# One block for every stage of an attention, cosine-layer and gated-layer kernel, with bias tiles copied straight from the staging buffer

## The chip, the cores and the metric

The kernel runs on one core of a Trainium2 chip. The metric is the device time of one execution in microseconds (us). Before the change it is 1207.83 us, the median of three runs from 1207.55 to 1208.03. The core's engines run their own instruction streams and meet at semaphores: PE (TensorE, matmuls; its weight loads are shown as PEld), DVE (VectorE), ACT (ScalarE), POOL (GpSimd) and SP (SyncE), which here only starts DMA transfers.

## The reference

```python
# attention over (batch 4, heads 8, seq 576, head_dim 64)
scores = q @ k.T / sqrt(64)
x = (log1p(|i - j|) / log1p(max(i, 1)))[..., None]
bias = relu(x @ w1 + b1) @ w2          # hidden 32, one value per head
attn = softmax(scores + bias);  a = attn @ v
x = a.transpose(0, 2, 1, 3).reshape(2304, 512)
h = x @ w_in;  x = (h * cos(h)) @ w_out                  # d_ff 2048
xn = x / sqrt(mean(x * x) + 1e-6) * rms_g
out = (silu(xn @ w_gate) * (xn @ w_val)) @ w_out2         # d_ff 1536
```

All data are float32. The bias depends on the position and the head only, so it is computed once (8 x 576 x 576) and used by all four batches.

## The kernel before

The program has four stages, and each is a `with nc.Block() as block:` of its own. At the end of a block all engines meet before any of them starts the next block.

**Bias stage** (`bias_phase`, lines 71 to 281). There are 12 rounds (`N`), and a round makes 3 groups (`KINDS`) of 16 rows for all 8 heads. ACT and DVE make the hidden values, PE multiplies them into the banks `bias_ps`, ACT writes the result into one of two sets of staging buffers (line 183, `stage_out`), and SP stores each group to a scratch tensor in DRAM (line 148). After 10 rounds SP loads the first three bias tiles of attention back from there (line 323). The staging of a later round waits until the store of the round two before it has landed.

**Attention stage** (`attention_phase`). There are 16 pairs of heads, numbered 0 to 15 here. A pair has 10 tiles of queries, five for each of its two heads, called s0 to s9; s4 and s9 have 64 rows, the others 128. One bias tile is held for each s; a new set is loaded every four pairs. In a slot PE makes the scores of a tile (line 506), turns an earlier tile (lines 528 and 532) and at slots 3, 5, 8 and 0 runs a quarter of the mix with the values (lines 546 and 552). The scores of a tile wait for the DVE's result on the tile two before it. DVE adds the bias and takes the maximum (line 644), ACT takes the exponential (line 594) and copies turned tiles, DVE and POOL share the normalising (line 412), and POOL splits q and k of the next pair in a high and a low part. In the last pair POOL splits the weight units 0 to 2 of the next layer in its place, and units 3 to 7 after it (lines 777 and 782). At the stage's start SP loads the other seven bias tiles. At its end PE runs the mix of pair 15's first half, then the first chunk `first_h` of the cosine layer, whose inputs DVE and ACT split just then (`features.high`, `features.low`, lines 803 to 812), and then the mix of the second half.

**Cosine layer** (`cos_layer_phase`). Six tiles of 384 tokens, each with 16 chunks f. An `up` and a `down` are 12 matmuls each; `down(f)` follows `up(f+2)`. The chain of a chunk is: ACT line 1080 (`turns`), DVE lines 1116, 1121 and 1126, ACT line 1094 (sine), DVE line 1133 (product), ACT line 1066 (high part), POOL line 1184 (low part). In the first tile DVE and POOL also split two weight units per chunk, of f = 0 to 11, beginning with units 8 and 9. These go to the space that attention's tensors had. At the stage's start POOL sets constants, among them an identity matrix.

**Gated layer** (`gated_layer_phase`). Again six tiles, with 12 chunks of two `up` and one `down`. Its first gate and value are made at the end of the cosine layer.

Every engine runs its stream in order, so an instruction that waits holds back all that stands behind it.

Of the kernel before, what the change touches and what calls it, by code (L numbers as in the profile page):

```python
# [35 lines left out]
EARLY_TILES = 3  # L36

# [4 lines left out]
LAG1, LAG2 = 3, 2  # L42
UNIT = KC * P
# [27 lines left out]
def bias_phase(nc, sb, sem_of, ins, bias_scratch, att):  # L71
# [36 lines left out]
    bias_staged = [sem_of(f"p0_bias_staged{k}") for k in range(KINDS)]  # L108
    bias_stored = att.bias_stored
# [7 lines left out]
    assert N % 2 == 0 and EARLY % 2 == 0  # L117
# [10 lines left out]
    with nc.Block() as block:  # L128

        @block.sync  # L130
        def _(sp):
            sp.dma_start(table[:, :], ins["log_table"]).then_inc(table_in, 16)
            sp.dma_start(inv_psi[:, :], ins["inv_psi"]).then_inc(consts_in, 16)
            sp.dma_start(w1b1[:, :], ins["w1b1"]).then_inc(consts_in, 16)
            sp.dma_start(w2rep[:, :], ins["w2rep"]).then_inc(w2_in, 16)
            sp.wait_ge(w2_zero, 1)
            for g in range(GR):
                sp.dma_start(w2blk[g * HID:(g + 1) * HID, g, :], ins["w2"]).then_inc(w2_in, 16)
            for h in range(2):
                att.load_qk(sp, 0, h, True)  # L140
            att.load_values(sp, 0, 0, True)
            att.load_values(sp, 1, 1, True)

            def store(m):
                for n, parity in ((m * 2, 0), (m * 2 + 1, 1)):
                    for k in range(KINDS):
                        sp.wait_ge(bias_staged[k], n + 1)
                        sp.dma_start(scratch[bass.ds(n * (KINDS * ROWS) + k * ROWS, ROWS), :, :],
                                     stage[parity][k][:, :, :].rearrange("p a b -> p (a b)")
                                     ).then_inc(bias_stored[parity][k], 16)  # L150


            with sp.Fori(0, EARLY // 4) as m:
                store(m)
            for h in range(2):
                att.load_qk(sp, 1, h, False)
            with sp.Fori(EARLY // 4, EARLY // 2 + 1) as m:
                store(m)
            for stored in (*bias_stored[0], *bias_stored[1]):
                sp.wait_ge(stored, 8 * EARLY)  # L160
            for s in range(EARLY_TILES):
                att.load_bias(sp, 0, s, True, 0)
            with sp.Fori(EARLY // 2 + 1, N // 2) as m:
                store(m)

        @block.gpsimd
        def _(pool):
            pool.memset(w2blk[:, :, :], 0.0).then_inc(w2_zero, 1)
            pool.memset(shift[0][:, :], 0.0).then_inc(shift_zero, 1)
            att.setup(pool)  # L170
            att.prepare(pool, 0, 0)
            att.prepare(pool, 0, 1)

        @block.scalar
        def _(act):
            act.wait_ge(slope_ready, 2)
            act.wait_ge(table_in, 16)

            def stage_out(n, parity, k, first):
                act.wait_ge(bias_summed[k], n + 1)  # L180
                if not first:
                    act.wait_ge(bias_stored[parity][k], (n - parity) * 8)
                act.activation(stage[parity][k][:, :, :], bias_ps[k][:, :, 0:HS], ACT.Identity, bias=shift[min(k, 1)][:, :],
                               scale=float(D) ** 0.5).then_inc(bias_staged[k], 1)

            def groups(n, parity, step):

                for j in range(ACT_STEPS[0]):
                    if step > 1 and j == 0:
                        act.wait_ge(bias_summed[0], n - 1)  # L190
                    act.activation(hidden[parity][0][j][:, :], table_window(n, 0, j), ACT.Relu, bias=b1c,
                                   scale=slope_of(n, 0, j)).then_inc(act_hidden[0], 1)
                    if step > 0:
                        stage_out(n - 1, 1 - parity, j, step <= 2)

            groups(0, 0, 0)
            act.wait_ge(shift_ready, 2)
            groups(1, 1, 1)
            groups(2, 0, 2)
            groups(3, 1, 3)  # L200
            with act.Fori(2, N // 2) as m:
                groups(m * 2, 0, 3)
                groups(m * 2 + 1, 1, 3)
            for k in range(KINDS):
                stage_out(N - 1, 1, k, False)

        @block.vector
        def _(dve):
            dve.wait_ge(consts_in, 16 * 2)
            dve.tensor_scalar(neg_b1[:, :], b1c, -1.0, None, ALU.mult).then_inc(slope_ready, 1)  # L210
            dve.tensor_scalar(slope[:, :], inv_psi[:, :], w1c, None, ALU.mult).then_inc(slope_ready, 1)
            dve.wait_ge(slope_ready, 2)
            dve.wait_ge(table_in, 16)
# [155 lines left out]
def attention_phase(nc, sb, sem_of, att, features, weights, chunks, bank_pairs, banks):  # L369
# [45 lines left out]
    with nc.Block() as block:  # L415

        @block.sync
        def _(sp):
# [20 lines left out]
            for w in range(RAW):  # L439
                weights.load(sp, w)  # L440
# [1042 lines left out]
```

## Time and profile before

| | |
|---|---|
| median of three runs | 1207.83 us (1207.55 to 1208.03) |
| the profiled execution: its time, its span | 1208.74 us, 1207.0 us |
| PE busy | 1171.1 us, 97% of the span |
| PEld, DVE, ACT, POOL busy | 1078.6, 704.4, 496.3, 490.4 us |
| mean granted PE clock | 0.996 of full speed |
| DMA | 69.06 MB, 57 GB/s over the span |

In the 40 slices of the page PE is at 9 (90% or more) in nearly all, and at 5, 7 and 8 in the first three. A busy PE in this profile need not be at its peak, since the ends of its matmuls are modelled; that is why gaps between starts are read as well. The bias stage runs to about 66 us, attention from 68 to 341 us, the cosine layer to 755 us and the gated layer to the end.

### The profile page before, as it was taken

The page shows a single profiled execution, that of the slowest core. Times are in us where ns is not written, and L with a number is a line of the kernel's source. Part 1 is how long each engine was busy: PE and PEld are TensorE (multiplying, and loading weights), DVE is VectorE, ACT ScalarE, POOL GpSimd, SP SyncE. Part 2 cuts the span into 40 slices and gives each one's busy share as a digit, 9 for nine tenths or more (in the row PEclk, how much of TensorE's full clock was granted, in tenths as well). Part 3 has the DMA queues.
Part 4 walks back from the last instruction along what each step waited for, and adds up shares of the span by engine and source line. Part 5 has one row for each costly group of instructions (what it writes and reads, how often), then busy time and mean ns, then how long its engine had stood idle before and what let it go on. Part 6 is the DMA issues. An engine that isn't in the chain of part 4 may idle for free. (4 is left out here: it accounts for less than half of the span.)

```text
span 1207.0 us, 21829 instructions
## 1 busy us (share of the span) xinstructions
PE 1171.1 (97%) x7464; PEld 1078.6 (89%) x7464; DVE 704.4 (58%) x1540; ACT 496.3 (41%) x1034; POOL 490.4 (41%) x515
## 2 busy tenths in 40 slices
PE   5789999999989999999999999999999999999998
PEld 2267777777779999999999999999999999999998
DVE  8978888888889867777786887553011020210201
ACT  6967787787723433333343333111111111111111
POOL 3047777777766342525243362751111111111111
PEclk9989999999999999999999999999999999999999
DMA  5754535252144000000000011330000000000000
GB/s 172 247 174 126 170 99 170 100 188 81 56 114 123 18 2 1 0 0 0 0 0 0 0 36 35 105 114 27 1 1 26 0 26 0 0 26 0 26 0 26
DMA packets 46534, 69.06 MB, mean 57 GB/s; under 512 B 3712, under 2 KB 27424, under 8 KB 46496
## 3 DMA queue, kind: packets, MB, share of 16 engines
q1 hardware_dynamic: 46496, 68.60, 18.3%
q8 instruction: 19, 0.31, 0.1%
q14 instruction: 19, 0.16, 0.0%
HBM read 53.25 MB, written 15.34 MB: 57 GB/s over the span
## 5 line engine op out<-in xcount | busy, mean ns | idle before, releaser
L820 PE MATMUL banks<-x_high,w_low_rest 128*128 128x384 f32 x672 | 224.5, 334 | 0.0
L818 PE MATMUL banks<-x_high,w_high_rest 128*128 128x384 f32 x672 | 224.4, 334 | 0.0
L819 PE MATMUL banks<-x_low,w_high_rest 128*128 128x384 f32 x672 | 224.4, 334 | 0.0
L1367 DVE TENSOR_TENSOR X<-X,banks 128x384 f32<-128x384 f32 x72 | 39.8, 552 | 298.6 <-PE banks L820 298.5
L1386 POOL TENSOR_TENSOR product_low<-X,product_high 128x384 fp32r<-128x384 f32 x72 | 72.8, 1012 | 345.5 <-ACT product_high L1329 345.5
L1184 POOL TENSOR_TENSOR product_low<-g,product_high 128x384 fp32r<-128x384 f32 x96 | 102.3, 1066 | 236.9 <-ACT product_high L1066 236.9
L818 PE MATMUL bank<-product_high,w_high_rest 128*128 128x384 f32 x480 | 162.1, 338 | 0.8 <-POOL product_low L1184 0.8
L820 PE MATMUL bank<-product_high,w_low_rest 128*128 128x384 f32 x480 | 160.5, 334 | 0.0
L819 PE MATMUL bank<-product_low,w_high_rest 128*128 128x384 f32 x480 | 160.5, 334 | 0.0
L1094 ACT ACTIVATE angle<-angle,quarter 128x384 f32<-128x384 f32 x96 | 59.3, 617 | 201.9 <-DVE angle L1126 201.9
L644 DVE CUSTOM_DVE_ANT_0 probs<-banks,bias 128x576 f32<-128x576 f32 (+1 forms) x160 | 119.7, 748 | 20.6 <-PE banks L506 10.0
L594 ACT ACTIVATE probs<-probs,neg_max 128x576 f32<-128x576 f32 (+1 forms) x160 | 123.4, 771 | 9.2 <-DVE neg_max L644 7.9
L819 PEld LDWEIGHTS banks<-x_low,w_high_rest 128*128 128x128 f32 x672 | 126.1, 188 | 0.0
L818 PEld LDWEIGHTS banks<-x_high,w_high_rest 128*128 128x128 f32 x672 | 126.1, 188 | 0.0
L820 PEld LDWEIGHTS banks<-x_high,w_low_rest 128*128 128x128 f32 x672 | 126.1, 188 | 0.0
L506 PE MATMUL banks<-k_high,q_parts 128*128 128x288 f32 x320 | 108.9, 355 | 3.7 <-PEq L128 2.5
L1316 ACT ACTIVATE X<-banks 128x384 f32<-128x384 f32 x71 | 34.9, 492 | 183.4 <-PE banks L820 183.4
L1329 ACT ACTIVATE product_high<-X 128x384 fp32r<-128x384 f32 x72 | 37.8, 526 | 174.5 <-DVE X L1367 174.5
L608 ACT ACTIVATE probs_t<-bank 128x512 f32<-128x512 f32 (+1 forms) x160 | 87.2, 546 | 48.7 <-PE bank L532 48.7
L1121 DVE SCALAR_TENSOR_TENSOR angle<-turns,angle 128x384 f32<-128x384 int32 x96 | 105.4, 1098 | 3.1
L412 POOL TENSOR_SCALAR probs<-probs,inv_total 128x576 f32<-128x576 f32 (+1 forms) x80 | 59.5, 743 | 101.3 <-DVE inv_total L656 98.0
L818 PEld LDWEIGHTS bank<-product_high,w_high_rest 128*128 128x128 f32 x480 | 90.1, 188 | 2.1 <-POOL product_low L1184 1.1
(113 smaller groups left out, 2525.4 us busy)
## 6 DMA issues: line engine op xcount, KB each, us to landing
raw_qk<-in_qk SPq DMA_DIRECT2D x32, 576.0 KB, 3.8
bias_scratch<-bias_stage SPq DMA_DIRECT2D x36, 288.0 KB, 3.2
bias<-bias_scratch SPq DMA_DIRECT2D x32, 288.0 KB, 3.4
w_raw<-in_w_out SPq DMA_DIRECT2D x28, 256.0 KB, 2.7
values<-in_v SPq DMA_DIRECT2D x16, 320.0 KB, 4.1
w_raw<-in_w_in SPq DMA_DIRECT2D x16, 256.0 KB, 2.9
out_t<-X SPq DMA_DIRECT2D x5, 768.0 KB, 3.6
w_raw<-in_w_gate SPq DMA_DIRECT2D x12, 256.0 KB, 3.3
```

Source lines behind the costliest of these rows:

```text
L412: eng.tensor_scalar(probs[s][0:rows], probs[s][0:rows], inv_total[0:rows, s:s + 1], scalar2, ALU.mult, op1).then_inc(normed, 1)
L506: last = nc.tensor.matmul(scores[s % 2][:, half, 0:HS], att.q_parts[h][:, qt * P:(qt + 1) * P], k_part[:, half * HS:(half + 1) * HS], star ...
L594: act.activation(probs[s][0:rows], probs[s][0:rows], ACT.Exp, bias=neg_max[0:rows, s:s + 1], scale=-1.0, accum_out=total[0:rows, s:s + 1]) ...
L608: act.activation(probs_t[parity][:, h, :, qt * P:qt * P + rows], turned[s % 2][:, 0:(NQ - 1) * rows].rearrange("p (c q) -> p c q", c=NQ - ...
L644: dve.tensor_tensor_reduce(out=probs[s][0:rows], in0=scores[s % 2][0:rows, :, 0:HS], in1=bias[s][0:rows, :, :], scale=-float(D) ** -0.5, s ...
L818: nc.tensor.matmul(out, high, x_high, start=start, stop=False)
L819: nc.tensor.matmul(out, high, x_low, start=False, stop=False)
L820: return nc.tensor.matmul(out, low, x_high, start=False, stop=stop)
L1094: act.activation(angle[:, :], angle[:, :], ACT.Sin, bias=quarter[:, :]).then_inc(cos_ready, 1)
L1121: dve.scalar_tensor_tensor(angle[:, :], turns[:, :], -TWO_PI_LOW, angle[:, :], ALU.mult, ALU.add).then_inc(fine_angle, 1)
L1184: pool.tensor_tensor(gl[f % 2][:, :], g[:, :], gh[f % 2][:, :].bitcast(F32), ALU.subtract).then_inc(g_split, 1)
L1386: pool.tensor_tensor(sl[f % 2][:, :], s, sh[f % 2][:, :].bitcast(F32), ALU.subtract).then_inc(s_split, 1)
```

## The change

One `nc.Block()` is opened in `build`, and all stages add their code to it. Waits on semaphores stand where the ends of the blocks stood. Beside that:

- The eight rounds before the last four are stored as before. In the last four (`DIRECT_ROUNDS`) SP also copies each group's rows of heads 0 and 1 from the staging buffer into their bias tiles, two more transfers of 16 rows for each group. Six bias tiles (s0 to s2, s5 to s7) are loaded from the scratch tensor after round 8's transfers, and the load of the other four for the first pairs is gone.
- PE's first scores wait for the last staging of their banks, and DVE's first tile for the last staging of all.
- In pairs 14 and 15 DVE and ACT split the inputs of the first token tile. In attention's tail PE runs the first two chunks' `up` between the turns, then both halves of the last mix, the second in the bank of `turned_end`. ACT loads the sine table ahead of its last copies and takes `turns` of chunk 0 ahead of the last.
- POOL's order after its units 3 to 7 is the low part of chunk 0, a wait for the last mix, constants (two, the identity is kept from attention), then units 8 and 9. DVE takes the last two copies of the mix in the cosine layer's first chunk.

```diff
+        def store_and_copy(n, parity):
+            for k in range(KINDS):
+                store(n, parity, k)
+                qt, row = divmod(n * (KINDS * ROWS) + k * ROWS, P)
+                for h in range(2):
+                    sp.dma_start(att.bias[h * NQ + qt][row:row + ROWS, :, :].rearrange("p a b -> p (a b)"),
+                                 stage[parity][k][h:P:H, :, :].rearrange("p a b -> p (a b)")
+                                 ).then_inc(bias_direct[parity][k], 16)
...
+        with sp.Fori(EARLY // 4, EARLY // 2) as m:
+            store_rounds(m)
+        store_and_copy(EARLY, 0)
         for stored in (*bias_stored[0], *bias_stored[1]):
             sp.wait_ge(stored, 8 * EARLY)
-        for s in range(EARLY_TILES):
+        for s in range(TILES):
+            if s % NQ < EARLY_TILES:
                 att.load_bias(sp, 0, s, True, 0)
+        store_and_copy(EARLY + 1, 1)
+        store_and_copy(EARLY + 2, 0)
+        store_and_copy(EARLY + 3, 1)
...
+            if copied:
+                act.wait_ge(bias_direct[parity][k], 2 * 16)
...
-            for s in range(MIX_SLOTS[1] + 1):
-                slot(PAIRS, 0, s, 2, compute=False)
-            pe.wait_ge(biased, PAIRS * TILES)
-            chunks.first_h(pe)
+        for s in range(T_LAG):
+            if s == MIX_SLOTS[3]:
+                mix(LAST - 1, 0, 1, 1, False)
+            turn(LAST, TILES - T_LAG + s, False)
+            if s == 0:
+                pe.wait_ge(biased, PAIRS * TILES)
+                chunks.first_h(pe, 0)
+            elif s == 2:
+                chunks.first_h(pe, 1)
+        for half in range(2):
             for part in range(2):
-                mix(LAST, 1, 1, part, False)
+                mix(LAST, 1, half, part, False, att.mixed_end if half else mixed)
...
+        def early_features(s, parts):
+            k = parts[0] if s < NQ else parts[1]
+            if s % NQ == 2 and k in DVE_PARTS:
+                dve.wait_ge(mixed_copied, (k * B + 1) * 2)
+                features.high(dve, 0, k)
+            elif s % NQ == 4:
+                features.low(dve, 0, 0, k)
...
+        pair(LAST - 1, 0, 2, made=lambda s: early_features(s, (0, 1)))
+        pair(LAST, 1, 2, made=lambda s: early_features(s, (2, 3)))
...
+                if first and f == 0:
+                    att.keep_mixed(dve, PAIRS - 1, 0)
+                    product(t, f, first)
+                    att.keep_mixed(dve, PAIRS - 1, 1, att.mixed_end)
...
+                if first and f == 0:
+                    low_part(t, f)
+                    pool.wait_ge(att.mixed_ready, PAIRS * 2)
+                    norm.setup(pool)
```

## Rows read from the trace of the kernel before

**Rows 1.** Waits of PE from 60 us on: total us, times, longest us.
```profile
PE banks L818 <- DVE x_low L812: 2.7, 7, 0.8
PE banks L506 <- PEq L128: 2.5, 1, 2.5
```
**Rows 2.** Windows: length, busy us (x instructions) of each engine, PEclk, DMA share, GB/s.
```profile
core 0: us, PE busy (x) PEld busy (x) DVE busy (x) ACT busy (x) POOL busy (x), PEclk, DMA share, GB/s
20.00:24.00 4.00, 4.00 (x40) 1.73 (x44) 3.85 (x8) 1.67 (x3) 0.00 (x0) 0.59 0.29 78
66.00:76.00 10.00, 7.97 (x36) 7.30 (x37) 6.00 (x21) 5.02 (x13) 2.08 (x4) 0.66 0.71 232
294.00:310.00 16.00, 16.00 (x121) 12.45 (x120) 13.42 (x46) 12.56 (x32) 12.22 (x14) 1.00 0.26 94
850.00:1000.00 150.00, 150.00 (x866) 150.00 (x865) 22.41 (x44) 26.30 (x52) 24.17 (x25) 1.00 0.03 11
```
**Rows 3.** Timeline of ACT, bias stage: start, us, line, [idle before]; first and last of 12.
```profile
49.39 0.74 ACT L183 ACTIVATE bias_stage<-bias_ps,shift 128x576 f32<-128x576 f32 x1
...
65.61 0.74 ACT L183 ACTIVATE bias_stage<-bias_ps,shift 128x576 f32<-128x576 f32 x1 [1.22 <-PE bias_ps L253]
```
**Rows 4.** Timeline of SP: bursts of bias loads.
```profile
58.64 1.35 SPq L323 DMA_DIRECT2D bias<-bias_scratch  x3
...
69.98 4.17 SPq L323 DMA_DIRECT2D bias<-bias_scratch  x7
```
**Rows 5.** Line 148, the bias stores: issue ns min/median/max; us to landing.
```profile
L148 SPq DMA_DIRECT2D bias_scratch<-bias_stage x36: 538/549/721, 12.5 to 66.4; - x36
...
DMA to landing us min/median/max: 3.0/3.2/6.3
```
**Rows 6.** Line 323, the bias loads: issue ns min/median/max.
```profile
L323 SPq DMA_DIRECT2D bias<-bias_scratch x40: 332/333/1134, 58.6 to 261.3; - x40
```
**Rows 7.** Timeline of DVE, pair 0: s4 and s6.
```profile
74.11 0.75 DVE L644 CUSTOM_DVE_ANT_0 probs<-banks,bias 64x576 f32<-64x576 f32 x1
...
77.62 0.76 DVE L644 CUSTOM_DVE_ANT_0 probs<-banks,bias 128x576 f32<-128x576 f32 x1 [0.94 <-DMA bias<-bias_scratch]
```
**Rows 8.** Timeline of PE: the first scores.
```profile
67.99 0.58 PE L506 MATMUL banks<-k_high,q_parts 128*128 128x288 f32 x1 [2.45 <-PEq L128]
```
**Rows 9.** Timeline of PE, from the tail of attention into the cosine layer.
```profile
334.01 0.41 PE L818 MATMUL banks<-x_high,w_high_head 128*128 128x384 f32 x1 [0.73 <-DVE x_low L812]
...
340.05 0.75 PE L552 MATMUL bank<-probs_t_end,values 128*128 128x288 f32 x2
...
347.16 0.41 PE L818 MATMUL bank<-product_high,w_high_head 128*128 128x384 f32 x1 [1.13 <-POOL product_low L1184]
...
351.40 0.41 PE L818 MATMUL bank<-product_high,w_high_head 128*128 128x384 f32 x1
```
**Rows 10.** Timeline of POOL, the same stretch.
```profile
329.43 0.62 POOL L777 TENSOR_SCALAR w_high_head<-w_raw 128x512 fp32r<-128x512 f32 x1
...
331.38 0.72 POOL L777 TENSOR_SCALAR w_high_head<-w_raw 128x512 fp32r<-128x512 f32 x1
...
342.42 1.50 POOL L777 TENSOR_SCALAR w_high_rest<-w_raw 128x512 fp32r<-128x512 f32 x2
...
350.23 1.01 POOL L1184 TENSOR_TENSOR product_low<-g,product_high 128x384 fp32r<-128x384 f32 x1 [1.64 <-ACT product_high L1066]
```
**Rows 11.** Timeline of DVE, the same stretch.
```profile
332.23 4.94 DVE L812 TENSOR_TENSOR x_low<-X,x_high 128x384 fp32r<-128x384 f32 x4
...
345.90 0.55 DVE L1116 SCALAR_TENSOR_TENSOR angle<-turns,banks 128x384 f32<-128x384 int32 x1
...
348.04 1.09 DVE L782 TENSOR_TENSOR w_low_rest<-w_raw,w_high_rest 128x512 fp32r<-128x512 f32 x1
```
**Rows 12.** Line 812, low parts of the inputs: ns min/median/max.
```profile
L812 DVE TENSOR_TENSOR x_low<-X,x_high x48: 546/551/1628, 332.2 to 1125.3; 128x384 fp32r<-128x384 f32 x48
```
**Rows 13.** Timeline of PE where the cosine layer's block ends.
```profile
754.30 0.34 PE L820 MATMUL bank<-product_high,w_low_rest 128*128 128x384 f32 x1
755.11 0.41 PE L818 MATMUL banks<-x_high,w_high_head 128*128 128x384 f32 x1 [0.47 <-PEq L1006]
```

More of the change, by code:

```diff
@@ L36 @@
 EARLY_TILES = 3
+DIRECT_ROUNDS = 4
+DIRECT_OF_FOURTH = ((0, 0), (0, 1))
 NT = 384
@@ L1210, in cos_layer_phase, with gated_layer_phase @@
     ctx.close()
-def gated_layer_phase(nc, sb, sem_of, norm, features, weights, chunks, out_t):
+def gated_layer_phase(nc, block, sb, sem_of, norm, features, weights, chunks, out_t):
     ctx = ExitStack()
@@ new lines, in _, with store @@
+    @block.sync
+    def _(sp):
+        for w in range(U1 + AHEAD + RAW, U1 + U2):
+            weights.load(sp, w)
+        def store(t, home, parts):
+            sp.wait_ge(out_kept, t * KC + parts.stop)
+            sp.dma_start(out_t.rearrange("(k p) t -> p k t", p=P)[:, parts, bass.ds(t * NT, NT)],
+                         X3[:, parts, bass.ds(home * NT, NT)]).then_inc(out_stored, 16)
+        with sp.Fori(0, T - 1) as t:
+            store(t, t + 1, slice(0, KC))
+        store(T - 1, 0, slice(0, KC - 1))
+        store(T - 1, 0, slice(KC - 1, KC))
+        sp.wait_ge(out_stored, 16 * (T + 1))
@@ new lines, in _, with tile @@
+    @block.scalar
+    def _(act):
+        def tile(t, first, last):
+            for f in range(C2):
+                c1 = t * C2 + (f + 1)
+                if not (first and f == 0):
+                    act.wait_ge(gate_ready, c1)
+                    act.wait_ge(s_ready, c1 - 1)
+                    act.activation(silu, gate_ps[:, 0:NT], ACT.Silu).then_inc(silu_ready, 1)
+                if f == C2 - 1 and not last:
+                    act.wait_ge(val_ready, c1)
+                    for k in ACT_PARTS:
+                        features.high(act, t + 1, k)
+                act.wait_ge(s_ready, c1)
+                if f >= 2:
+                    act.wait_ge(down_done, t * DOWNS + (f - 1))
+                elif not first:
+                    if f == 0:
+                        act.wait_ge(down_done, t * DOWNS)
+                    else:
+                        act.wait_ge(out_ready, t * KC)
+                act.activation(sh[f % 2][:, :], s, ACT.Copy).then_inc(s_high, 1)
+        for d in norm.KEPT_BY_ACT:
+            norm.keep(act, T - 1, d)
+        tile(0, True, False)
+        act.wait_ge(norm.scaled, T * KC)
+        with act.Fori(1, T - 1) as t:
+            tile(t, False, False)
+        tile(T - 1, False, True)
```

1418 lines of the change are left out of this document (702 added, 716 removed).

## The prediction

> **What bounds the kernel now.** I read the page first: PE is busy for 1171.1 of 1207.0 us, so nothing but its 36 us of idle time, its low clock and its waits can be gained, and the change adds and removes no matmul. Second, the list of PE's waits: behind the bias stage the largest are 2.7 us on the low parts of the inputs of the first token tile and 2.5 us on the start of the attention block [rows 1]. Third, windows. In the middle of attention PE is busy for all of 16 us while DVE has 13.42 and POOL 12.22; in the layers 150 us hold 866 matmuls, 0.1732 us each or 4.16 us for a chunk of 24 [rows 2]. There PE sets the pace, so what is gained at an entrance arrives undiminished at the end. So I price three places: bias to attention, attention to cosine layer, cosine to gated layer.
>
> **Entrance to attention.** What goes: the last staging ends at 65.61 + 0.74 = 66.35 us [rows 3], yet PE starts its scores at 67.99, 2.45 us after the last bias matmul [rows 8]. DVE then meets a late bias load at s6, at 77.62, after 0.94 us of idle time, while s4 stood at 74.11 [rows 7]. Now PE starts behind its last bias matmul and DVE at 66.4. What comes in its place is SP's queue. Round 8's first staging ends at 49.39 + 0.74 = 50.13 [rows 3]. From there SP issues, per round, three stores and six copies. A store takes 0.549 us, with the gap 0.60 [rows 5]. A copy of 16 rows is not in the trace. The nearest rows are the bias loads: 0.333 us when the queue is idle, 0.38 with a gap [rows 6], 1.35 / 3 = 0.45 in the burst at 58.64, 4.17 / 7 = 0.60 in the burst at 69.98 [rows 4]. I take 0.45, the burst that lies between the same stores, and keep 0.38 and 0.60 as ends. A round is then 3 x 0.60 + 6 x 0.45 = 4.5 us, about ACT's own pace of 4.4 ((65.61 - 49.39) / 11 = 1.47 for a group [rows 3]), so SP never recovers what it falls behind. Behind round 8 stand six loads of tiles instead of three behind round 9, 6 x 0.45 = 2.7. Round 8 is issued at 54.6, the loads at 57.3, round 9 at 61.8, round 10 at 66.3, round 11 at 70.8. With 3.2 us from the start of an issue to landing [rows 5], less the 0.4 of the issue, the last copy is there at 73.6.
>
> Who waits for it: DVE's s4, which needs all copies (s3 needs round 10's first two groups, issued by 64.8). Left alone, DVE would reach s4 at about 66.4 + 4 x 1.28 = 71.5 (half of the 2.57 below per slot). So it waits to 73.6, and behind it stand the guards, inversions and all later tiles, and PE's score of s6, which waits for s4. From s4 to s6 it is 77.62 - 0.94 - 74.11 = 2.57 us without the old wait [rows 7]: s6 comes at 76.2 instead of 77.6, **1.45 us gained**, not the 3.1 that the start promises.
>
> PE's clock takes part of it. After 2.45 us of idle time the granted clock fell to the lower level: the mean is 0.66 over 66 to 76, so 6.8 us at 1.2 GHz, and 0.59 over 20 to 24, 3.3 us at that level [rows 2]. Before, those slow matmuls fell on slots 0 to 4, where there are few turns and DVE has time. Now PE runs dry after the scores of s5, at 71.6, until 74.4, and if the clock falls it is slots 5 to 9 that are slow, with a score and a turn each. Between nothing and 1.1 us, I take 0.55. Entrance: **0.9 us gained**; the ends are below.
>
> The Trainium skill, page "SBUF — State Buffer", section "The DMA setup-cost knee", has a fixed 2 us for a transfer, plus its bytes over the bandwidth; its table for 16 partitions gives about 104 GB/s, so a copy of 36 KB would land in 2.4 us rather than the 3.2 of a store. No transfer of that shape is in this trace. By the rule the last copy is there 0.8 us sooner and the sum below would be 3.6. Its advice to use 128 partitions and few transfers speaks against 24 small ones.
>
> **Pairs 14 and 15.** Two casts and two low parts come to pair 14, two low parts to pair 15, on DVE. A low part takes 0.551 us alone [rows 12] and 4.94 / 4 = 1.24 beside POOL's splits [rows 11]; a cast is bounded by the same two figures. Pair 14 gets 2.2 to 5.0 us and has 16 - 13.42 = 2.6 free [rows 2], pair 15 gets 1.1 to 2.5. PE's scores wait for the tile two before, so nearly all of it fits into the slack: 0.4 us on PE, from 0 to 2.4. What it certainly delays is pair 15's last inversion, by one low part of about 0.75 us, and with it POOL's last normalising and the weight units behind that.
>
> **Entrance to the cosine layer.** What goes: `first_h` started at 334.01 after a wait, was held up for want of inputs, 2.7 us in all [rows 1], and the last mix ended at 340.05 + 0.75 = 340.8; then came the block's end, two chunks' `up`, and a wait of 1.13 us for POOL, and `down(0)` started at 347.16 [rows 9]. In PE's own work `down(0)` could start 6 us sooner. But two chains stand in front.
>
> POOL: units 3 to 7 started at 329.43, one per 1.95 us where DVE did not disturb it (331.38 - 329.43) [rows 10]. They now start at 330.2 and end at 330.2 + 5 x 1.95 = 339.9. Only then comes the low part of chunk 0, 1.01 us [rows 10], to 341.0 (by 0.4 the later of the two; the last mix is over before that (340.8 before; one `up` more, 12 x 0.1732 = 2.08, the 2.7 us of waits less, 0.4 for the pairs: 340.6)), then two constants, 0.3, and unit 8's high part at 341.3 instead of 342.42 [rows 10].
>
> DVE: chunk 0 is done except the product long before, so it splits unit 8 when its high part is there (342.05, after 1.50 / 2 [rows 10]), 1.09 us beside POOL [rows 11], and unit 9 (0.551 x 512 / 384 = 0.73 alone [rows 12], less some overlap), and starts chunk 1 at **343.8 instead of 345.90** [rows 11]. From there a chunk takes 351.40 - 347.16 = 4.24 us [rows 9], more than PE's 4.16: DVE holds the pace in the first tile. So 2.1 us are gained, whatever PE could do.
>
> PE's new wait: `down(0)` at 341.3, `up(3)` done at 345.5, `down(1)` at 343.8 + (351.40 - 345.90) = 349.3 [rows 9, 11]. That is 3.8 us idle, longer than the 2.45 us that brought the clock down [rows 2, 8]. I expect 3.3 us of the lower level, the shorter of the two stretches, for back-to-back matmuls: half of it, 1.65, is lost. While PE is behind, it makes 0.08 per chunk good against DVE's 4.24, eleven chunks, 0.9. So 2.1 - 1.65 + 0.9 = 1.35; I take **1.3 us gained**.
>
> **Entrance to the gated layer.** 755.11 - 754.30 = 0.81 where 0.17 is the normal pitch [rows 13]: **0.64 us gained**; the work behind it has its inputs, as only the last `down` of the layer stands between. The kernel's end stays: the same stores, one block end.
>
> **Sum.** 0.9 + 1.3 + 0.64 = 2.8 us. The profiled execution took 1208.74 us with a span of 1207.0, so 1205.9 by its own time; the median of the runs is 0.9 lower, and I take the 2.8 from that: **1205.0 us**.
>
> **Rivals.**
> - *The covers hold.* Copies and loads issue at 0.38 [rows 6]: a round is 4.1, the loads 2.3, the last issue ends at 69.1, and with the shortest landing, 3.0 less 0.4 [rows 5], the last copy is there at 71.7, about when DVE needs it. s6 at 74.3, 3.3 us gained. No idle stretch of PE costs clock: 2.1 at the second entrance. With 0.64: 6.0 us, 1201.8. For it: the issue times with an idle queue. Against: DMA share is 0.71 over 66 to 76 already [rows 2], and the 3.8 us of idle time follow from POOL's and DVE's orders.
> - *Clock takes it all.* Both stalls cost 6.8 us of the lower level as after 66 [rows 2]. 1.45 - 1.05 = 0.4; 2.1 - 3.4 + 0.9 = -0.4; 0.64. 0.6 us gained, 1207.2: no change.
> - *SP's queue becomes the bound (slower).* Copies and loads issue at 0.60 [rows 4]: a round is 5.4, the loads 3.6; the rounds end at 55.5, then 59.1 for the loads, 64.5, 69.9 and 75.3, the last copy is there at 78.1, s6 at 80.7: 3.1 us lost. With 0.55 of clock and the other gains, 1.8 us slower, 1209.6; at the longest landing, 6.3 us [rows 5], 1212.7. It decides from a last copy later than 76.4.
> - *The change doesn't do what it says:* were the single block still to hold the engines up at the stage ends, s0 would come at 69.5 as before, and little beside the 2 us of the cosine layer would be left. It is part of the second case.
>
> **Chances.** What runs of this kernel can tell from no change is 0.2%, 2.4 us; the forecast lies just above it. Forecast 0.47, of which 0.33 above the 2.4 us and 0.14 below; covers hold 0.20; clock takes all 0.19, of which 0.18 are no change; SP's queue 0.14. Faster 0.53, within 0.32, slower 0.15. The range goes from the best case, with 0.4 less in the pairs, to SP's queue at 0.60 per issue: 1201.4 to 1209.5.
>
> **What would show it.** In the trace after: PE's first score right behind the last bias matmul near 65.6; DVE's s4 waiting for a transfer, near 73.6; the last direct copy issued near 70.8 (69 and less speaks for the first rival, 75 for the third). POOL's low part of chunk 0 straight behind unit 7, near 340; the first `angle` of chunk 1 near 343.8; PE idle for over 3 us before `down(1)`, and a granted clock below 1.00 in the 5 us behind it. No gap at the gated layer. The prediction is wrong if DVE never waits for the copies, if POOL isn't the last to arrive at the cosine layer, or if pairs 14 and 15 take over 1 us more than those before them.

## The result, and the profile after

| | median us | runs | lowest to highest |
|---|---|---|---|
| before | 1208.03 | 7 | 1207.55 to 1208.88 |
| after | 1212.11 | 7 | 1211.52 to 1213.29 |

The ratio is 1.0033, with a 95% interval of 1.0022 to 1.0044: the change makes the kernel about 4 us slower. The profiled execution after took 1212.11 us with a span of 1210.1; the one before had a span of 1207.0, so 3.1 us are to be found between the two traces.

The first step is to lay the traces side by side at instructions that both have. DVE's copies of finished results serve: the first one of attention, one near attention's end, and the last of the kernel. Before (start, us, engine, line):

```profile
92.38 0.46 DVE L665 COPY X<-bank 128x288 f32<-128x288 f32 x1 [0.78 <-PE bank L552]
...
320.95 0.46 DVE L665 COPY X<-bank 128x288 f32 x1 [0.67 <-PE bank L552]
...
1201.37 2.15 DVE L1344 COPY X<-bank 128x384 f32<-128x384 f32 x4 [2.52 <-PE bank L820]
```

and after:

```profile
96.24 0.46 DVE L357 COPY X<-bank 128x288 f32<-128x288 f32 x1 [0.78 <-PE bank L585]
...
325.23 0.43 DVE L357 COPY X<-bank 128x288 f32<-128x288 f32 x1
...
1204.52 2.14 DVE L1417 COPY X<-bank 128x384 f32<-128x384 f32 x4 [2.54 <-PE bank L872]
```

With two more marks, POOL's low part of chunk 1 (350.23 before [rows 10], 351.03 after) and PE's wait near the end of the cosine layer (746.04 and 748.76), and DVE's first addition of the gated layer (756.36 and 757.90), the 3.1 us come apart:

| stretch | start after minus start before | change in the stretch |
|---|---|---|
| up to attention's first copy | +3.86 | 3.86 lost |
| attention | +4.28 | 0.42 lost |
| tail and first cosine chunks | +0.80 | 3.48 gained |
| cosine layer | +2.72 | 1.92 lost |
| entrance to the gated layer | +1.54 | 1.18 gained |
| gated layer | +3.15 | 1.61 lost |

The last two rows depend on the mark. PE's first matmul of the gated layer stands at 755.11 before [rows 13] and at 757.22 after:

```profile
757.05 0.34 PE L872 MATMUL bank<-product_high,w_low_rest 128*128 128x384 f32 x1
757.22 0.33 PE L870 MATMUL banks<-x_high,w_high_head 128*128 128x384 f32 x1
```

By this mark, 2.11 apart, the entrance gained 0.61 and the gated layer lost 1.04.

Two things stand out. The entrance to attention went the wrong way. And both layers, whose code did not change, got longer, by 3.0 us together on PE.

**The entrance: SP's queue.** SP's timeline after, from round 8 on:

```profile
50.63 1.22 SPq L163 DMA_DIRECT2D bias<-bias_stage  x2
51.90 0.60 SPq L148 DMA_DIRECT2D bias_scratch<-bias_stage  x1
52.54 1.23 SPq L163 DMA_DIRECT2D bias<-bias_stage  x2
...
55.93 3.07 SPq L349 DMA_DIRECT2D bias<-bias_scratch  x6
59.05 0.58 SPq L148 DMA_DIRECT2D bias_scratch<-bias_stage  x1
...
74.70 0.60 SPq L148 DMA_DIRECT2D bias_scratch<-bias_stage  x1
75.34 1.23 SPq L163 DMA_DIRECT2D bias<-bias_stage  x2
```

A copy takes 0.60 us to issue, 0.64 with the gap, and a group of one store and two copies comes every 1.91 us (from 51.90 to 53.81, and to the end at the same pitch). ACT stages one every 1.47 [rows 3]. So SP falls behind, and from 55.93 on it never waits: the last copy is issued at 76.57. ACT's timeline shows the queue reaching back to it. The staging of round 11 has to wait until round 9's copies have read the buffer (the first two of them, issued from 59.67 behind the six loads, took 4.6 to 4.8 us to land; the last ones of all took 2.3 to 2.5):

```profile
60.98 0.74 ACT L202 ACTIVATE bias_stage<-bias_ps,shift 128x576 f32<-128x576 f32 x1
65.22 0.74 ACT L202 ACTIVATE bias_stage<-bias_ps,shift 128x576 f32<-128x576 f32 x1 [3.49 <-DMA bias<-bias_stage]
```

DVE's timeline: s4 waits for the last copies, and s6 comes 3.2 us later than before [rows 7], where 1.45 earlier was forecast.

```profile
78.53 0.75 DVE L684 CUSTOM_DVE_ANT_0 probs<-banks,bias 64x576 f32<-64x576 f32 x1 [6.40 <-DMA bias<-bias_stage]
...
80.82 0.76 DVE L684 CUSTOM_DVE_ANT_0 probs<-banks,bias 128x576 f32<-128x576 f32 x1
```

PE ran dry for 4.85 us before its next score at 79.34, and in the windows (columns as in [rows 2]) the granted clock is at 0.54 in the 5 us behind it, nearly all of them at the lower level, after it had been at 0.66 in the 5 us ahead of it; that it makes up the rest between the 3.2 us of s6 and the 3.86 of the first copy is likely, but was not tested.

```profile
70.00:75.00 5.00, 3.96 (x18) 3.39 (x16) 2.10 (x9) 2.60 (x7) 2.02 (x3) 0.66 0.71 189
75.00:80.00 5.00, 0.66 (x3) 0.66 (x4) 1.47 (x6) 0.68 (x1) 0.00 (x0) 0.77 0.36 107
80.00:85.00 5.00, 5.00 (x25) 4.62 (x25) 4.15 (x14) 4.28 (x12) 4.19 (x4) 0.54 0.01 3
```

**The layers: every matmul a little longer.** PE is busy for all of both windows, at a granted clock of 1.00. Before:

```profile
1000.00:1100.00 100.00, 100.00 (x578) 100.00 (x577) 13.42 (x26) 17.22 (x34) 16.16 (x17) 1.00 0.02 8
```

After:

```profile
1000.00:1100.00 100.00, 100.00 (x576) 100.00 (x575) 13.44 (x26) 17.20 (x34) 16.22 (x16) 1.00 0.02 8
```

Two matmuls fewer in 100 us, with DVE, ACT and POOL doing the same. The groups by line and form (busy us, mean ns of one) say which. A matmul's record reaches into the next one's: in the kernel before it is 334 ns long where the next starts 173.3 ns later. So these means order the groups, and the steps are read further down. Before:

```profile
L819 PE MATMUL banks<-x_low,w_high_rest 128*128 128x384 f32 x672 | 224.4, 334 | 0.0
L819 PE MATMUL bank<-product_low,w_high_head 128*128 128x384 f32 x144 | 48.1, 334 | 0.0
L819 PE MATMUL banks<-x_low,w_high_tail 128*128 128x384 f32 x48 | 16.3, 339 | 0.0
```

After:

```profile
L871 PE MATMUL banks<-x_low,w_high_rest 128*128 128x384 f32 x672 | 226.2, 337 | 0.0
L871 PE MATMUL bank<-product_low,w_high_head 128*128 128x384 f32 x144 | 48.6, 337 | 0.0
L871 PE MATMUL banks<-x_low,w_high_tail 128*128 128x384 f32 x48 | 16.1, 336 | 0.0
```

The rest and the products got slower, the tail faster. That is no matter of clock or waits. What else differs is where the buffers lie: the change puts `warm` (4 bytes, which take 32) ahead of the weights, so the rest of the weights starts 32 bytes further, and it moves the first product pair to the upper end of the memory. In the kernel before, head, rest, `x` and products all started 128 bytes past a multiple of 256, and only the tail, the one slow group, did not. (Addresses are worked out from the buffers' sizes in the order of allocation. No view prints them: how far a buffer moves from one kernel to the next follows from the code, the bytes past a multiple of 256 as such are not measured.)

### The profile page after: what moved, and what is told of

Same layout as the page of the kernel before. It is cut to its first block, busy times and chain, and to the rows that moved or that the text cites. A ratio compares the mean times of both kernels' runs of the same rounds, so it can differ in the third digit from the quotient of the medians.

```text
span 1210.1 us, 21703 instructions
## 1 busy us (share of the span) xinstructions
PE 1173.6 (97%) x7464; PEld 1084.1 (90%) x7464; DVE 704.9 (58%) x1540; ACT 496.2 (41%) x1034; POOL 491.2 (41%) x513
## 4 chain that ended last, share of the span: by engine, by line
PE 52%; issue 29%; DVE 7%; POOL 6%; SPq 2%; DMA 1%; ACT 1%; POOLq 0%; DVEq 0%; ACTq 0%
PE banks L537 7%; PE banks L870 6%; PE banks L872 6%; PE banks L871 6%; PE bank L579 5%; PE bank L870 5%; PE bank L872 5%; PE bank L871 5%; PE bank L563 5%; POOL product_low L1459 5%; PE bank L585 2%; DVE angle L1187 1%; SPq L163 1%; DVE w_low_rest L834 1%; DVE angle L1182 1%
## 5 line engine op out<-in xcount | busy, mean ns | idle before, releaser
L632 ACT ACTIVATE probs<-probs,neg_max 128x576 f32<-128x576 f32 (+1 forms) x160 | 123.3, 771 | 11.6 <-DVE neg_max L684 10.6
L563 PE MATMUL bank<-ident,probs 128*128 128x128 f32 (+1 forms) x640 | 92.5, 268 | 0.0
```

Source lines behind the costliest of these rows:

```text
L563: last = nc.tensor.transpose(turned[s % 2][:, c * rows:(c + 1) * rows], flat[0:rows, at:at + P], ident[0:rows, 0:rows])
L632: act.activation(probs[s][0:rows], probs[s][0:rows], ACT.Exp, bias=neg_max[0:rows, s:s + 1], scale=-1.0, accum_out=total[0:rows, s:s + 1]) ...
```

## Experiments at the entrance

**No copies.** The changed kernel, SP only storing, and s3, s4, s8, s9 loaded from the scratch once all stores have landed:

```
-        store_and_copy(EARLY + 1, 1) ... (EARLY + 3, 1)
+        store_rounds(EARLY // 2 + 1)
...
+        for s in range(TILES):
+            if s % NQ >= EARLY_TILES:
+                att.load_bias(sp, 0, s, True, 0)
```

> The changed kernel without the direct copies: SP stores all twelve rounds, and loads the bias tiles s3, s4, s8 and s9 from the scratch when all stores have landed, in the one block. Theory S (SP's queue, 24 copies at 0.61 us, is what held ACT and DVE up): stagings end near 65.5 us again, DVE's s4 starts at about 73.5, s6 at about 77, so attention runs 3.5 to 4 us earlier than in the changed kernel: 1208.3 beside 1212.1. Theory T (the copies only show a cost of the one block, or of the traffic in this stretch): s6 stays behind 79, under 1.5 us gained.

Measured: 1209.14 us, 3.0 less than the changed kernel, ratio to before 1.0015 (1.0006 to 1.0024). Stagings end at 66.1. DVE waits at s3, to 73.97, s4 is at 74.95, s6 at 78.14, 2.7 us ahead of the changed kernel; attention's first copy comes at 92.94. Theory S gets its places within 1.5 us and its time within 0.9; theory T is out.

**Few copies.** Only round 10's last group and round 11 go straight, and the copies come ahead of the last round's stores. s3 and s8 are loaded. Every engine that writes where the staging buffers were now waits for the last stores.

```
+        copy(EARLY + 2, 0, 2)
+        copy(EARLY + 3, 1, 0)
+        (wait for all stores up to round 10, group 1)
+        att.load_bias(sp, 0, EARLY_TILES, True, 0)
+        copy(EARLY + 3, 1, 1)
+        copy(EARLY + 3, 1, 2)
+        att.load_bias(sp, 0, NQ + EARLY_TILES, True, 0)
+        for k in range(KINDS):
+            store(EARLY + 3, 1, k)
```

> The changed kernel with 8 direct copies instead of 24: only the rows of s4 and s9 go straight (round 10 k 2, round 11), issued ahead of the last round's stores; s3 and s8 are loaded from the scratch when round 10 has landed. The buffers' readers wait for the last stores. Theory S: SP never falls behind ACT (round 10 takes five issues, 3.0 us of 4.4; round 11's six copies end near 69), stagings end at 65.5, DVE's s4 starts at 71.5 to 72.5 and s6 at about 74.5, 3 us ahead of the kernel before and 6 of the changed one: 1206 beside 1212.1 (the layers as in the changed kernel). Theory T: s6 behind 78, at least 1210.

Measured: 1204.30 us, 7.8 less than the changed kernel; ratio to before 0.9969 (0.9957 to 0.9981). DVE's timeline has no wait at s3 (69.26), s4 or s6:

```profile
70.35 0.75 DVE L697 CUSTOM_DVE_ANT_0 probs<-banks,bias 64x576 f32<-64x576 f32 x1
...
72.83 0.76 DVE L697 CUSTOM_DVE_ANT_0 probs<-banks,bias 128x576 f32<-128x576 f32 x1
```

s6 stands 4.8 us ahead of the kernel before, where 3 were expected, and the time is 1.7 us under the expected 1206. SP's timeline ends its copies at 68.5:

```profile
62.08 3.14 SPq L161 DMA_DIRECT2D bias<-bias_stage  x4
65.70 0.34 SPq L358 DMA_DIRECT2D bias<-bias_scratch  x1
66.10 2.39 SPq L161 DMA_DIRECT2D bias<-bias_stage  x4
68.54 0.58 SPq L358 DMA_DIRECT2D bias<-bias_scratch  x1
```

A third of the copies does all that the 24 were to do: the rows of the earlier rounds came through the scratch in time. The edit also puts the last copies ahead of the last stores, and what that alone is worth was not separated.

**Copies on POOL's queue.**

```
-                    sp.dma_start(att.bias[h * NQ + qt][row:row + ROWS, ...
+                    pool.dma_start(att.bias[h * NQ + qt][row:row + ROWS, ...
```

> The changed kernel with all 24 direct copies issued from POOL's queue, which is idle then, and the stores left on SP's; the buffers' readers wait for the last stores. Theory S (the bound is how many DMAs one queue issues, 0.6 us each): SP's rounds take 1.8 to 2 us again, stagings end near 65.5 us, DVE's s4 starts at 72 to 74 us unless POOL takes over 0.73 us for one issue (six per 4.4 us round); 1205 to 1207 beside 1212.1. Theory L (what is slow is the landing of these 16-row copies whoever issues them): s4 stays at 78 us, 1212.

Measured: 1213.52 us, ratio to before 1.0041 (1.0026 to 1.0057). The time alone looks like theory L. The timelines of POOL, of DVE and of ACT tell otherwise:

```profile
50.52 13.70 POOL L185 DMA_DIRECT2D bias<-bias_stage  x1 [33.05 <-ACT bias_stage L208]
...
72.83 0.49 POOL L185 DMA_DIRECT2D bias<-bias_stage  x1
```

```profile
59.63 2.53 DVE L250 TENSOR_SCALAR hidden<-log_table,slope,neg_b 128x576 f32 x5
62.09 2.04 DVE L250 TENSOR_SCALAR hidden_last<-log_table,slope,neg_b 128x576 f32 x4
```

```profile
66.16 0.74 ACT L208 ACTIVATE bias_stage<-bias_ps,shift 128x576 f32<-128x576 f32 x1 [8.06 <-DMA bias<-bias_stage]
```

POOL's first copy took 13.70 us to issue, to 64.22. DVE worked without a gap on the hidden rows until 62.09 + 2.04 = 64.13, which were its last of the stage, and ACT's staging stood still for the copies. The median of all 24 issues is 0.487 us, less than SP's. So the bound was not POOL's usual issue time, which I had allowed for, but one issue that ended 0.09 us after DVE's last instruction. Not every instruction of DVE holds POOL up: two copies from 75.75 on took 0.96 us together while DVE was at s0 and s1 (75.56 to 76.99).

The Trainium skill's page "SBUF — State Buffer" has this in its section "SBUF: two separate sides": descriptors of a DMA from POOL are written through a port pair that a DVE instruction in a 2-port mode holds for itself. The trace agrees as far as it goes, with 13.7 us for the first and 0.49 for one with DVE idle, but it does not show the mode of DVE's instructions, and that the first copy on POOL's queue is slow by itself was not tested.

This run therefore does not separate S from L as it was meant to. The landing times do it better: in the changed kernel the 24 copies have a minimum of 2.3 and a median of 2.5 us from issue to landing, against 3.2 for a store; only the four behind the six loads took longer, 3.6 to 4.8, and s4 does not hang on those. So the copies are not slow to land, and s4 follows SP's last issue (76.57) by 1.96 us.

The 2.5 us agree with the 2.4 that the prediction estimated from the Trainium skill's page "SBUF — State Buffer", section "The DMA setup-cost knee". What failed in the sum was the issue: the list of line 163 has 586, 597 and 874 ns as minimum, median and maximum for the 24 copies.

## Experiments on the layers

**Rest back onto a multiple of 64.**

```
-        self.warm = sb(top, "warm", [P, 1], F32)
+        self.warm = sb(top, "warm", [P, 16], F32)
```

> The changed kernel with one buffer grown: warm is 64 bytes of each partition instead of 4 (which take 32), so that w_high_rest and w_low_rest, and the second pair of product buffers, start on a multiple of 64 bytes again, as in the kernel before; the units of the tail then don't. Theory A (a matmul whose operand starts 32 bytes off takes some 0.6 ns longer per issue): 36 matmuls of the gated layer take 6.24 us again instead of 6.26 to 6.27, the layers get back 2.3 us of the 2.6 they lost, about 1209.7 us beside 1212.1. Theory B (the layers are slower because their code now stands in one block with all else): no change, 1212.1. Theory C (the difference is one of executions, not of kernels): no change of the medians.

Measured: 1212.75 us, nothing regained. In its first form theory A is wrong.

**The kernel before, shifted by 32 bytes.**

```
+        sb(top, "pad", [P, 1], F32)
         weights.add_rest(sb, top)
```

> The kernel before with an unused buffer of 32 bytes allocated ahead of the layers' weights, nothing else: w_high_rest, w_low_rest and both pairs of product buffers start 32 bytes off a multiple of 64, the tail's units come onto one. Theory A: 2 to 3 us slower, 1210.5 beside 1208.0, the gated layer's 36 matmuls at 6.26 us or more. Theories B and C: 1208.0.

Measured: 1211.69 us beside 1207.84; ratio 1.0035 (1.0022 to 1.0049). An unused buffer of 32 bytes costs the kernel before 3.9 us. That ends theories B and C: it has no new block and no new code.

**Which operand.** The same unused bytes put behind the rest, so that only the products move, or on both sides of it, so that the products move by 128 in all and the weights by 32 or 64:

```
         weights.add_rest(sb, top)
+        sb(top, "pad", [P, 1], F32)      # e6; [P, 32] in e12
```

```
+        sb(top, "pad", [P, 1], F32)      # e7; [P, 16] in e11
         weights.add_rest(sb, top)
+        sb(top, "pad2", [P, 24], F32)    # e7; [P, 16] in e11
```

> The kernel before with 32 unused bytes between the rest of the weights and the product buffers: only the products (32 off a multiple of 128) and what lies above them move; the weights of rest and head, and x, stay on one. Theory A' with the moving operand as the cause: the groups with products at 175 ns or more, those with x at 173.4. With the weights as the cause, or only both together: all at 173.4, and about 1207.5 (the tail comes onto a multiple of 64).

> The kernel before with 32 unused bytes ahead of the rest of the weights and 96 behind it: only the weights of rest stand 32 off a multiple of 128, the products stay on one. With the weights as the cause: the groups of rest at 174.5 or more whatever they move, those of head at 173.4; about 1210. With the moving operand as the cause: 1208, all at 173.4.

> The kernel before with 64 unused bytes ahead of the rest of the weights and 64 behind it: only the weights of rest move, onto a multiple of 64 that is none of 128; the products stay on 128, as in e7 with 32. If a multiple of 64 is enough: 1207.9, the groups of rest at 173.4 ns. If it takes 128: the groups of rest at 174.3 ns or more, 1210 or more, in e1 those with x took 174.3 to 174.5 there.

> The kernel before with 128 unused bytes between the rest of the weights and the product buffers: all large buffers of the layers but the tail stay on multiples of 128, but in the kernel before (and in e5 and e10) every one of them stood 128 past a multiple of 256, and now the products stand on one. Theory A' (any multiple of 128 is as good): 1208, groups with products at 173.4 ns. Theory A'' (what counts is where weight and moving operand stand to each other within 256 bytes; in e7 and e11 the head's weights, not moved, took 176.5 ns with products that had come onto a multiple of 256): the 1870 matmuls of head and rest with products take 176.5 ns, 3.1 more, 5.8 us in all, 1213 to 1214; those with x stay at 173.4.

Measured, with ratios to before: e6 1208.51 us (1.0005, 0.9995 to 1.0014), e7 1213.79 (1.0047, 1.0032 to 1.0063), e11 1212.31 (1.0032, 1.0020 to 1.0044), e12 1213.20 (1.0045, 1.0029 to 1.0062). The step from one matmul's start to the next, as a mean over 870 to 1170 us of each trace, by what is moved (x or product) and which weights stand (ns; the numbers in brackets are the bytes past a multiple of 256, weights and then moving operand):

| kernel | x, head | x, rest | x, tail | product, head | product, rest | product, tail |
|---|---|---|---|---|---|---|
| before | 173.3 (128, 128) | 173.3 (128, 128) | 176.7 (32, 128) | 173.3 (128, 128) | 173.3 (128, 128) | 176.6 (32, 128) |
| after | 174.2 (128, 128) | 173.8 (160, 128) | 173.3 (64, 128) | 175.0 (128, 224 and 160) | 174.5 (160, 224 and 160) | 175.1 (64, 224 and 160) |
| e1 | 173.9 (128, 128) | 174.3 (192, 128) | 176.8 (96, 128) | 174.9 (128, 224 and 192) | 173.5 (192, 224 and 192) | 176.2 (96, 224 and 192) |
| e2 | 174.2 (128, 128) | 173.8 (160, 128) | 173.3 (64, 128) | 173.3 (128, 160) | 175.6 (160, 160) | 176.6 (64, 160) |
| e6 | 174.2 (128, 128) | 173.6 (128, 128) | 173.1 (64, 128) | 173.2 (128, 160) | 173.3 (128, 160) | 176.6 (64, 160) |
| e7 | 173.7 (128, 128) | 174.0 (160, 128) | 174.0 (160, 128) | 176.4 (128, 0) | 176.4 (160, 0) | 175.9 (160, 0) |
| e11 | 173.6 (128, 128) | 174.8 (192, 128) | 173.4 (160, 128) | 176.4 (128, 0) | 173.6 (192, 0) | 175.9 (160, 0) |
| e12 | 173.6 (128, 128) | 173.5 (128, 128) | 174.0 (160, 128) | 176.4 (128, 0) | 176.4 (128, 0) | 175.9 (160, 0) |

The same pair of numbers gives steps within 0.9 ns of each other: (128, 0) is 176.4 each time, (32, 128) is 176.7 and 176.6, (64, 128) is 173.1 to 173.3, but (128, 128) is 173.3 to 174.2. The slowest and the fastest lie 3.7 ns apart, 2%. e6 speaks against the moving operand as the cause, since the products moved and stayed at 173.2 and 173.3 with head and rest. e7 fits neither of its theories: the weights of rest moved, yet with x they took 174.0, and the products took 176.4 with the head's weights, which had not moved. In e7 the products had come onto a multiple of 256, and e12 is the clean case for that. There nothing moved but the products, by 128 bytes, and what lies behind them, the tail included. The groups by line and form of e12:

```profile
L819 PE MATMUL banks<-x_low,w_high_rest 128*128 128x384 f32 x672 | 224.9, 335 | 0.0
L819 PE MATMUL bank<-product_low,w_high_rest 128*128 128x384 f32 x480 | 162.3, 338 | 0.0
L819 PE MATMUL bank<-product_low,w_high_head 128*128 128x384 f32 x144 | 48.7, 338 | 0.0
```

338 ns with products, 335 with x, on the same weights: 5.3 us for the kernel, where 5.8 were expected. So it is neither the weights' address nor the products' alone but the two together, and a multiple of 128 is not enough; theory A' is out, A'' stands as far as it goes. A part of it is no matter of the pair at all but of the change from one group to the next. With the first six matmuls after each change of group taken apart from those that follow, x with the head's weights in e6 has 176.8 and then 173.3 ns, x with the weights of rest in the changed kernel 175.1 and then 173.4, and the pair (160, 160) of e2 177.9 and then 173.3. So (160, 160) costs nothing once it runs, like (128, 128). Others stay slow: (128, 0) at 176.0 to 176.1, (32, 128) at 176.2 to 176.6, (192, 128) at 174.4 to 174.8. With all on 128 (e5 and e10, below) both parts are at 173.3. I have no rule that gives these numbers, nor is it shown what in the chip does this.

**All as in the kernel before, tail included.** `warm` and `quarter` share 96 bytes at the upper end, and 96 unused bytes stand ahead of the tail. Every large buffer of the layers then starts 128 past a multiple of 256.

```
-        self.warm = sb(top, "warm", [P, 1], F32)
+        self.edge = sb(top, "edge", [P, 24], F32, "right")
+        self.warm = self.edge[:, 0:1]
...
-        self.quarter = sb(ctx, "quarter", [P, 1], F32, "right")
+            chunks.quarter = att.edge[:, 1:2]
...
+        sb(top, "pad", [P, 24], F32)
         cos_layer_phase(...)
```

In the kernel with few copies:

> The kernel of e4_few_copies with every large buffer moved onto a multiple of 128 bytes of its partition: warm and quarter share 96 bytes at the upper end, and 96 unused bytes stand ahead of the tail's units. Nothing else differs. Theory A' (the mean from one matmul of the layers to the next depends on where both operands start; in the kernel before, head, rest, x and the products all start on multiples of 128 and take 173.3 to 173.7 ns, its tail 32 bytes off one takes 176): every group falls to 173.3 to 173.5 ns, tail included; 2250 matmuls of the cosine layer gain 1.1 ns each and 2050 of the gated layer 0.8, 4.1 us in all: 1200.2 beside 1204.3. Theory D (the addresses matter only by the accident of which buffers meet in one moment, and there is no such multiple): some groups faster, some slower, within 1.5 us of 1204.3.

Measured: **1200.49 us**, 3.8 less than with few copies alone; ratio to before 0.9939 (0.9925 to 0.9952). Every group of the gated layer is at 173.3 ns, the tail too:

```profile
L886 PE MATMUL banks<-x_low,w_high_rest 128*128 128x384 f32 x672 | 224.4, 334 | 0.0
L886 PE MATMUL bank<-product_low,w_high_head 128*128 128x384 f32 x144 | 48.1, 334 | 0.0
L886 PE MATMUL banks<-x_low,w_high_tail 128*128 128x384 f32 x48 | 16.0, 334 | 0.0
```

The expectation had this of any multiple of 128, and it came true by luck: all of them happened to be 128 past a multiple of 256, and e12 showed afterwards that this matters. Not all of the difference between the two traces is the addresses': PE waited 2.16 us for chunk 1 in the one with few copies and the granted clock fell, 1.79 us here and it did not, and from POOL's low part of chunk 1 to that of chunk 15 the first took 59.76 us and the second 58.92. That is 0.8 of the 5.1 us between the two spans; the medians lie 3.8 apart.

In the changed kernel itself:

> The changed kernel with every large buffer on a multiple of 128 bytes, and nothing else. If the two causes add up: 3.8 us less, as between e4 and e5, 1208.3 beside 1212.1, and level with the kernel before.

Measured: 1208.85 us, 3.3 less than the changed kernel, ratio to before 1.0004 (0.9995 to 1.0013). The two causes add up within 0.6 us: 7.8 and 3.3 one by one, 11.6 together (1212.11 to 1200.49).

## An experiment on the tail

`up` of chunk 1 behind the last mix again, in the kernel with few copies:

```
-FIRST_H = 2
+FIRST_H = 1
...
-            elif s == 2:
-                chunks.first_h(pe, 1)
```

> The kernel of e4_few_copies with one chunk computed in attention's tail instead of two (FIRST_H = 1): up(1) runs behind the last mix. If PE's idle time behind the last mix is all slack, since POOL's splits and DVE's split low parts set chunk 1 (rough at 339.8 us while the mixes end at 335.9): no change, 1204.3. If up(1)'s 2.1 us were on the path: up to 2.1 slower. My own prediction had PE idle for 3.8 us there and at half clock after it: with up(1) moved into the gap the idle time falls by 2.1 us, so if that idle time cost clock it would now cost less, up to 0.9 us faster.

Measured: 1206.31 us, 2.0 more than e4; ratio to before 0.9986 (0.9977 to 0.9995). PE's slack did not cover it, by a way that I had not thought of: ACT's order has the turns of chunk 1 ahead of the high part of chunk 0, so ACT waited 4.72 us for the later `up`, POOL's low part of chunk 0 came at 337.41 instead of 335.90, and all behind it 1.5 us later, which is the difference of the two spans (1204.5 and 1203.0). So it is the order on ACT that gives the second early chunk this worth; that another order would take it away was not tested. One further execution of this kernel took 5316.51 us; it has no trace, its cause is not known, and the ratio leaves it out.

## Why the prediction was wrong

The forecast was 1205.0 us, the range 1201.4 to 1209.5, with 0.15 on slower. The time is 1212.11. By its steps:

- *PE and DVE start behind the bias stage* was right in kind: PE's first score waits for no block any more, only for ACT's last staging of the banks that it writes (66.10 against 67.99).
- *A copy issues in 0.45 us* is the step that failed. It took 0.60, 0.64 with the gap. I had taken the 0.45 of the burst between the stores and kept the 0.60 of the later burst as an end. With 0.60 the prediction's own third rival gives a last copy at 78.1 and s6 at 80.7; measured are 78.5 (s4's start) and 80.82. That rival was right in mechanism and place, and got 0.14. That its size at the entrance fits so well is in part luck: its issues were too fast (0.60 where a copy took 0.64 with the gap) and its landing too slow (3.2 where 2.5 were measured), and the two nearly cancel. Its time, 1209.6, was short by 2.5 us, since it too had nothing for the layers; its own case of the longest landing, 1212.7, was left out of the stated range. What should have moved the chance: even at 0.45 a round of SP (4.5) was longer than one of ACT (4.4), so the end of the queue lay behind the need in every case but the best.
- *From issue to landing* was put at 3.2 us for a copy and measured at 2.5; by this the last copy comes 0.7 earlier, and it is the one part of the entrance that was too dark.
- *Clock at the entrance*: 0.55 us from 0 to 1.1 was taken; 3.86 lost at the first copy against 3.20 at s6 leaves 0.66.
- *Pairs 14 and 15*: 0.4 us forecast. At DVE's copy of a result in pair 13 the two traces stand 3.99 us apart (288.35 and 292.34), at the one near the end of pair 15 4.04 (328.77 and 332.81), so the two pairs cost 0.05, the best case of the forecast. Of the 0.42 of all attention 0.13 came before, and the rest is the mark at 325.23, which stands late by itself; by the copy after it the tail gained 3.2 us, not 3.5.
- *Entrance to the cosine layer*: 1.3 us forecast, 3.48 measured. DVE's start of chunk 1 was right: 347.63 is 1.73 later than before, with attention 4.28 later, so 2.55 gained, where 2.1 stood. Two terms were wrong. The clock loss of 1.65 less 0.9 did not come: PE waited 1.97 us for the low part, not 3.8, and the granted clock was 1.00 in every window of 5 us from 325 to 360. And chunk 1 went faster than its pace. DVE's timeline after:

```profile
347.63 0.54 DVE L1182 SCALAR_TENSOR_TENSOR angle<-turns,banks 128x384 f32<-128x384 int32 x1
348.20 0.56 DVE L1187 SCALAR_TENSOR_TENSOR angle<-turns,angle 128x384 f32<-128x384 int32 x1
348.80 0.36 DVE L1192 TENSOR_SCALAR angle<-angle 128x384 f32<-128x384 f32 x1
```

  In the kernel before the second and third took 0.94 and 0.66. POOL stood still for 1.56 us there, waiting for a weight unit:

```profile
349.75 0.62 POOL L829 TENSOR_SCALAR w_high_rest<-w_raw 128x512 fp32r<-128x512 f32 x1 [1.56 <-DMA w_raw<-in_w_out]
351.03 1.00 POOL L1255 TENSOR_TENSOR product_low<-g,product_high 128x384 fp32r<-128x384 f32 x1 [0.67 <-ACT product_high L1134]
```

  From the first row of the chunk on DVE to POOL's low part it is 3.40 us instead of 4.33, and 2.55 + 0.93 = 3.48.
- *Entrance to the gated layer*: 0.64 forecast, 0.61 measured by PE's own mark, and PE's gap is gone (757.05 to 757.22 is the normal step). The 1.18 of the table has DVE's first addition for its mark. In the kernel before, DVE's last copies of the cosine layer waited for the end of the block; now two of the three run ahead of PE's first matmul of the gated layer, so this addition comes earlier against PE's work, and nothing shows that it moves PE.
- *"What is gained at an entrance arrives undiminished at the end"* is the assumption that failed outside the sum. The layers lost 3.0 us on PE (1.92 and 1.04), which no part of the prediction priced, since the code of the layers stood as it was; what the experiments show in its place is the buffers' addresses. e10, with nothing but addresses changed, gives 3.3 us back, a part of it by the tail's weights, which were slow in the kernel before too.

With the measured stages and no loss in the layers, the 3.1 us between the traces less 3.0 come out near no change, as e10 does. So the sign was decided by both causes: the queue ate what the tail gave, and the addresses made the result slower.

The stage sizes have an uncertainty of their own. Attention's first copy stands at 96.24, 95.60 and 97.12 in three traces (after, e1, e10) whose entrance is the same code, and at 92.38 and 91.56 in those of the kernel before and of e2; so the first row of the table is good to about 1 us.

## What to carry to other kernels

Count the DMAs that a change puts on one queue against the pace of the engine that feeds it, at the slowest issue time that any burst of the trace shows; if that is longer than the pace, the last transfer is as late as the whole sum, and it is better to send directly only what would be late than everything. Where a change adds, drops or reorders a buffer, look at where the large operands of the dense matmuls come to lie, and compare the mean time of the same group of matmuls before and after: 32 bytes cost this kernel 3.9 us, and putting all its operands back, the tail too, was worth 3.3 and 3.8 us.

## What was not expected of the hardware

- With fp32r operands of 384 columns, the mean step from one matmul to the next was 173.1 to 176.8 ns at a granted clock of 1.00, by where weights and moving operand start within 256 bytes and by where those of the group before do. The Trainium skill's page "SBUF — State Buffer", section "Operand start alignment", asks only that an operand start at a multiple of its element size and says that this is about legality, not speed; all placements here are legal, and they differ by 2%.
- A plain copy of 16 rows took 0.60 us to issue on SP, while a load of a whole tile took 0.51 in the same stretch (3.07 / 6) and 0.33 at the median. On POOL the same copy took 0.49 with DVE idle, and one took 13.7 us while DVE worked without a gap on the hidden rows.
- DVE's `TENSOR_SCALAR` on 128x384 took 0.36 us while POOL waited and 0.66 beside POOL's work, and the `SCALAR_TENSOR_TENSOR` ahead of it 0.56 and 0.94: here an engine's wait for data went with a faster neighbour.
- At one place, PE's wait ahead of chunk 1's `down`, small differences decided about the clock. After 1.68 (e10), 1.79 (e5), 1.97 (the changed kernel), 1.99 (e8) and 2.00 us (e3) of it the granted clock was 1.00 over the next 5 us; after 2.16 (e4), 2.52 (e1) and 2.81 us (e9) it was 0.66 to 0.68. The chunks from 1 to 15 took 59.8 us in e4, with the lower clock, and 59.0 in the changed kernel.
